# The order in which TensorE takes the columns of a matmul: groups of eight in place of groups of four, and the first block in that order too

## The chip, the cores and the metric

The kernel runs on one core of one Trainium2 chip. The metric is the device time of one execution in microseconds. Smaller is better.

## The reference, cut to what matters

Two sequences of 6080 tokens with 256 channels go through a gated scan and then through a feed-forward pair of products with an ELU between them.

```python
sig = 1 / (1 + exp(-f_logit))
f = lower_bound + (1 - lower_bound) * sig
for t in range(S):                       # S = 6080, for both batches
    h = f[:, t] * h + (1 - f[:, t]) * x[:, t]
    y[:, t] = h
hid = y.reshape(B * S, 256) @ w_in       # 256 -> 2048
g = where(hid > 0, hid, exp(min(hid, 0)) - 1)
out = g @ w_out                          # 2048 -> 256
```

All inputs and the output are float32.

## The kernel before, in words

**Layout.** Channels lie on the 128 partitions, tokens along the columns. The tokens of a sequence are cut into 12 blocks: block 0 has 448 columns (`SHORT`), blocks 1 to 11 have 512 (`TILE`). Both sequences are worked on in each block.

**Precision.** Each float32 operand is split into a rounded part and a rest, both of type float32r (`_hi`, `_lo`). Each product of two matrices is then three matmuls: hi with hi, hi with lo, lo with hi (lines 866 to 868 for the first layer, 897 to 899 for the second, 1002 to 1004 for the first layer in block 0).

**Work of TensorE.** In blocks 1 to 11 the first layer is done in seven products for each pair of hidden tiles instead of eight (a Strassen-like scheme; `P1` to `P7`, written out in `whole`, line 905). For each of the 8 pairs (`q`) a block has 7 products of three matmuls and 8 half tiles of the second layer of three matmuls: 45 matmuls, 360 in a block, 3960 in the eleven blocks. Block 0 uses the plain form: 32 tiles (`FIRST_TILES`), each with 6 matmuls of the first layer and 6 of the second, 384 in all. Before it stand 18 warm-up matmuls on bf16 zeros (line 1010). TensorE's queue is `first_products` (the first six tiles of block 0, line 961), then `first_product(t)` and `second(0, t - 6)` in turn (line 1012), then `whole` for each block.

**The other engines.** For each tile of the hidden layer ScalarE computes a negated relu of the bank (line 466) and an exponential (line 472), VectorE forms the ELU from the bank and that (line 719), ScalarE rounds it into `g_hi` (line 480), and GpSimd forms `g_lo` (line 336). The matmuls of the first layer write PSUM banks `h`; a bank is written again when the ELU of the tile before it in that bank is done (line 994 waits for `g_ready`). In blocks from 1 on ScalarE copies a bank (`fork`, line 458) and VectorE adds banks (lines 698, 705, 713) between products. The scan of the next block (lines 620, 628) and the splits of the weights in block 0 lie between these, in an order written out by hand (`spare`, `first_spare`, `early`, `late`). The SP queue loads and stores. Matmul number `t` of block 0's second layer comes six tiles after its first layer.

**The order of columns.** The function `in_order` (line 56) turns a view of the columns into four passes: the columns are cut into groups of `LINE` neighbours, and pass number a takes groups a, a + 4, a + 8 and so on (`APART` = 4). Output, moving operand and their partner in the product get the same order, so each column's result stands where it stood. `product` (line 860) uses it for every matmul of the first layer in blocks 1 to 11, `second` (line 870) for those of the second layer unless the block is block 0 (line 895). In block 0, `first_products` (lines 969, 976, 979, 983) and `first_product` (lines 1000 to 1004) read and write their columns in plain order. With `LINE` = 4 a pass over 512 columns is 32 groups of 4 columns (16 bytes) that start 16 columns (64 bytes) apart.

Of the kernel before, what the change touches and what calls it, by code (L numbers as in the profile page):

```python
# [21 lines left out]
SHORT = SEQ - (BLOCKS - 1) * TILE  # L22
# [5 lines left out]

EDGE = 8

LINE = 4
APART = 4

WIDE = 1
# [2 lines left out]
P1, P2, P3, P5, P6, P7, P4 = range(7)  # L37
# [15 lines left out]
PLACE = ((P1, P2), (P5, P4))  # L53


def in_order(columns):

    return columns.rearrange("p (b a c) -> p a b c", a=APART, c=LINE)


def width(j):
    return SHORT if isinstance(j, int) and j == 0 else TILE
# [18 lines left out]
def gated_scan_elu_ffn(nc, first_gate, forget_logit, value, w_in, w_out, out):  # L81
    ctx = ExitStack()
    with ctx:
# [51 lines left out]
        h = ctx.enter_context(nc.psum_tensor("h", [P, 4, TILE], F32))  # L135
# [50 lines left out]
        def first_bank(t):  # L186
            k = FIRST_BANK[t]
            return h[:, k] if k < TILES else acc[:, 1, k - TILES]
# [10 lines left out]
        def a_parts(par, product):  # L199
            if product == P4:  # L200
                return a4_hi[:, :], a4_lo[:, :]
            k = product
            return a_hi[:, par, k], a_lo[:, par, k]
# [655 lines left out]
        def _(pe):  # L859
# [10 lines left out]
            def second(j, t, half):  # L870

                w = width(j)
                first = isinstance(j, int) and j == 0
                if first:
                    b, unit = FIRST_TILES[t]
                    opens = unit == 0
                else:
                    b, unit = TILE_OF[t % TILES][0], 2 * (t // TILES) + TILE_OF[t % TILES][1]
                    opens = unit == b
                q, u = divmod(unit, 2)  # L880
                closes = unit == UNITS - 1 - b
                if half == 0:
                    if first:
                        pe.wait_ge(w_out_lo_ready[q], 1)
                    if opens and first and b == 1:

                        pe.wait_ge(g_ready, max(k for k in range(TILES * PAIRS) if FIRST_BANK[k] >= TILES) + 1)
                    if opens and not first:
                        pe.wait_ge(acc_copied, BATCH * HALVES * (j - 1) + HALVES * (b + 1))
                    pe.wait_ge(g_lo_ready, TILES * PAIRS * j + t + 1)  # L890
                cols = slice(half * P, (half + 1) * P)
                hi, lo = w_out_hi[:, q, u, cols], w_out_lo[:, q, u, cols]
                bank = acc[:, b, half, 0:w]
                g_h, g_l = g_hi[:, t % RING, 0:w], g_lo[:, t % RING, 0:w]
                if not first:
                    bank, g_h, g_l = in_order(bank), in_order(g_h), in_order(g_l)
                nc.tensor.matmul(bank, hi, g_h, start=opens, stop=False)  # L897
                nc.tensor.matmul(bank, hi, g_l, start=False, stop=False)  # L898
                done = nc.tensor.matmul(bank, lo, g_h, start=False, stop=closes)  # L899
                if half == 1:  # L900
                    done.then_inc(mm2_done, 1)
                elif closes:
                    done.then_inc(acc_half, 1)

            def whole(j, par):
                def m(q, back, i, half):

                    at = q - back
                    if at >= 0:
                        second(j, TILES * at + i, half)  # L910
                    else:
                        second(j - 1, TILES * (PAIRS + at) + i, half)
# [43 lines left out]
            def plain_weights(unit, half):  # L956
                p, u = divmod(unit, 2)
                k = QUARTER[half][u]
                return w_in_hi[:, p, k], w_plain_low[p][:, k]

            def first_products():

                pieces = [a_parts(0, PLACE[0][i]) for i in range(HALVES)]
                pe.wait_ge(zeros_ready, 3)
                for half in range(HALVES):
                    pe.wait_ge(a_hi_ready, half + 1)
                    for unit in range(OPEN):
                        pe.wait_ge(w_plain_hi_ready, unit // 2 + 1)
                        nc.tensor.matmul(first_bank(unit), plain_weights(unit, half)[0],  # L969
                                         pieces[half][0], start=half == 0, stop=False)  # L970
                for unit in range(OPEN):
                    w = TILE if unit < WIDE else SHORT
                    bank = first_bank(unit)[:, 0:w]
                    if unit == 0:
                        pe.wait_ge(a_lo_ready[P1], 1)
                    nc.tensor.matmul(bank, plain_weights(unit, 0)[0], pieces[0][1][:, 0:w], start=False, stop=False)
                    pe.wait_ge(w_plain_lo_ready[unit // 2], 1)
                    for half in range(HALVES):
                        nc.tensor.matmul(bank, plain_weights(unit, half)[1], pieces[half][0][:, 0:w],  # L979
                                         start=False, stop=False)  # L980
                    if unit == 0:
                        pe.wait_ge(a_lo_ready[P2], 1)
                    done = nc.tensor.matmul(bank, plain_weights(unit, 1)[0], pieces[1][1][:, 0:w],
                                            start=False, stop=True)
                    done.then_inc(done_of[unit % TILES], 1)

            def first_product(t):
                b, unit = FIRST_TILES[t]
                bank = first_bank(t)[:, 0:SHORT]
                pe.wait_ge(w_plain_lo_ready[unit // 2], 1)  # L990
                earlier = [k + 1 for k in range(t) if FIRST_BANK[k] == FIRST_BANK[t]]
                if earlier:
                    pe.wait_ge(g_ready, earlier[-1])
                for half in range(HALVES):
                    pe.wait_ge(a_lo_ready[PLACE[b][half]], 1)
                    hi, lo = plain_weights(unit, half)
                    a_h, a_l = [part[:, 0:SHORT] for part in a_parts(0, PLACE[b][half])]
                    if t == TILES * PAIRS - 2 and half == 0:

                        nc.tensor.matmul(h[:, 3], hi, a_parts(0, P5)[0], start=True, stop=False)  # L1000
                    else:
                        nc.tensor.matmul(bank, hi, a_h, start=half == 0, stop=False)  # L1002
                    nc.tensor.matmul(bank, hi, a_l, start=False, stop=False)  # L1003
                    done = nc.tensor.matmul(bank, lo, a_h, start=False, stop=half == 1)  # L1004
                done.then_inc(done_of[t % TILES], 1)
# [3 lines left out]
            for k in range(WARM_UP):  # L1009
                nc.tensor.matmul(h[:, k % 4, :], zeros[:, 0:P], zeros[:, 0:TILE], start=True, stop=True)  # L1010
            first_products()
            for t in range(OPEN, TILES * PAIRS):
                first_product(t)
                if t >= LEAD:
                    for half in range(HALVES):
                        second(0, t - LEAD, half)
# [46 lines left out]
```

## Time and profile before

| what | value |
|---|---|
| median of 3 runs | 976.56 us (976.37 to 976.63) |
| the profiled execution's own time | 976.51 us |
| its span (first to last instruction) | 974.6 us |
| TensorE matmul busy | 969.0 us, 99% |
| VectorE busy | 724.4 us, 74% |
| ScalarE busy | 790.7 us, 81% |
| GpSimd busy | 630.6 us, 65% |
| granted TensorE clock | full in every slice |
| chain that ended last | TensorE 99% |

The profile's duration of one matmul (about 384 ns at 512 columns) is longer than the time from its start to the start of the next, since matmuls are pipelined. The rate of TensorE is therefore read from the distance of starts, called the pace below.

### The profile page before, as it was taken

Reading aid. Unit: us, or ns where it says so; the run is one execution under the profiler, and the core shown is the slowest. Engines: PE = TensorE matmul, PEld = TensorE weight load, DVE = VectorE, ACT = ScalarE, POOL = GpSimd, SP = SyncE. Lnnn points to the kernel's source line nnn. Section 1 sums busy time; section 2 is a strip of 40 time slices with the busy share of each in tenths; the row PEclk is TensorE's granted clock in tenths of the full one; section 3 lists DMA queues with packets and bytes.
Section 4 is the critical chain, followed back from the end, with each engine's and each line's share of the span. In section 5 each row is a group of like instructions: output and inputs, shape, how many; then the busy total and the mean of one; then the engine's idle time right before and its main releaser. Section 6 shows DMA issues by size and latency. Waiting matters only on the chain.

```text
span 974.6 us, 15016 instructions
## 1 busy us (share of the span) xinstructions
PE 969.0 (99%) x4362; PEld 815.1 (84%) x4362; DVE 724.4 (74%) x916; ACT 790.7 (81%) x1424; POOL 630.6 (65%) x477
## 2 busy tenths in 40 slices
PE   9999999999999999999999999999999999999998
PEld 6998888888888888888888888888888888888887
DVE  6987876976886796697688679678758867956444
ACT  7988878878888887887887888788788788787775
POOL 2587796576667667557656755856775765676544
PEclk9999999999999999999999999999999999999999
DMA  7212012002101201100210210120021021001001
GB/s 269 67 32 93 0 34 65 34 1 77 54 1 54 76 1 43 54 32 2 74 54 0 65 65 0 45 67 17 22 64 43 0 75 54 0 0 46 1 1 44
DMA packets 23078, 42.02 MB, mean 43 GB/s; under 512 B 2560, under 2 KB 4096, under 8 KB 23040
## 3 DMA queue, kind: packets, MB, share of 16 engines
q1 hardware_dynamic: 22752, 41.10, 13.1%
q10 hardware_dynamic: 288, 0.46, 0.2%
q8 instruction: 18, 0.29, 0.1%
q14 instruction: 20, 0.16, 0.1%
HBM read 29.10 MB, written 12.45 MB: 43 GB/s over the span
## 4 chain that ended last, share of the span: by engine, by line
PE 99%; DMA 0%; DVE 0%; ACT 0%; issue 0%; DVEq 0%
PE acc L898 17%; PE acc L897 17%; PE acc L899 17%; PE h L868 14%; PE h L867 14%; PE h L866 14%; PE h L1004 1%; PE h L1003 1%; PE h L1002 1%; DMA opening<-first_gate 0%; PE h L969 0%; PE h L979 0%; PE acc L1002 0%; PE acc L1003 0%; PE acc L1004 0%; DVE x L628 0%
## 5 line engine op out<-in xcount | busy, mean ns | idle before, releaser
L336 POOL TENSOR_TENSOR g_lo<-e,g_hi 128x512 fp32r<-128x512 f32 (+1 forms) x384 | 517.3, 1357 | 338.0 <-ACT g_hi L480 337.0
L466 ACT ACTIVATE e<-h 128x512 f32<-128x512 f32 (+1 forms) x379 | 225.1, 594 | 138.5 <-PE h L868 109.9
L719 DVE SCALAR_TENSOR_TENSOR e<-e,h 128x512 f32<-128x512 f32 (+1 forms) x379 | 256.6, 677 | 70.5 <-ACT e L472 69.8
L897 PE MATMUL acc<-g_hi,w_out_hi 128*128 128x512 f32 (+1 forms) x768 | 293.7, 382 | 0.0
L898 PE MATMUL acc<-g_lo,w_out_hi 128*128 128x512 f32 (+1 forms) x768 | 293.7, 382 | 0.0
L899 PE MATMUL acc<-g_hi,w_out_lo 128*128 128x512 f32 (+1 forms) x768 | 293.7, 382 | 0.0
L472 ACT ACTIVATE e<-e 128x512 f32<-128x512 f32 (+1 forms) x384 | 241.4, 629 | 9.8 <-issue 1.4
L480 ACT CAST g_hi<-e 128x512 fp32r<-128x512 f32 (+1 forms) x384 | 232.2, 605 | 18.3 <-DVE e L719 18.3
L866 PE MATMUL h<-a_hi,w_in_hi 128*128 128x512 f32 x616 | 236.6, 384 | 0.0
L868 PE MATMUL h<-a_hi,w_in_lo 128*128 128x512 f32 x616 | 236.6, 384 | 0.0
L867 PE MATMUL h<-a_lo,w_in_hi 128*128 128x512 f32 x616 | 236.5, 384 | 0.0
L897 PEld LDWEIGHTS acc<-g_hi,w_out_hi 128*128 128x128 f32 x768 | 143.8, 187 | 26.5
L899 PEld LDWEIGHTS acc<-g_hi,w_out_lo 128*128 128x128 f32 x768 | 143.8, 187 | 26.5
L898 PEld LDWEIGHTS acc<-g_lo,w_out_hi 128*128 128x128 f32 x768 | 143.8, 187 | 26.5
L868 PEld LDWEIGHTS h<-a_hi,w_in_lo 128*128 128x128 f32 x616 | 115.3, 187 | 22.3
L867 PEld LDWEIGHTS h<-a_lo,w_in_hi 128*128 128x128 f32 x616 | 115.3, 187 | 22.2
L866 PEld LDWEIGHTS h<-a_hi,w_in_hi 128*128 128x128 f32 x616 | 115.3, 187 | 22.2
L713 DVE TENSOR_TENSOR h<-p,h 128x512 f32<-128x512 f32 x88 | 61.0, 693 | 73.0 <-PE h L868 72.8
L628 DVE TENSOR_TENSOR_SCAN x<-opening,carry,x 128x512 f32<-128x512 f32 (+1 forms) x48 | 102.2, 2129 | 0.1
L698 DVE COPY p<-h 128x512 f32<-128x512 f32 x88 | 59.7, 679 | 47.4 <-PE h L868 47.2
L705 DVE TENSOR_TENSOR h<-p,h 128x512 f32<-128x512 f32 x88 | 60.7, 690 | 34.9 <-PE h L868 33.9
L620 DVE SCALAR_TENSOR_TENSOR x<-opening,x 128x512 f32<-128x512 f32 (+1 forms) x48 | 56.3, 1172 | 0.1
(77 smaller groups left out, 560.3 us busy)
## 6 DMA issues: line engine op xcount, KB each, us to landing
opening<-forget_logit SPq DMA_DIRECT2D x44, 256.0 KB, 2.6
x<-value SPq DMA_DIRECT2D x44, 256.0 KB, 2.7
out<-out_sb SPq DMA_DIRECT2D x44, 256.0 KB, 2.0
w_in_raw<-w_in SPq DMA_DIRECT2D x8, 256.0 KB, 5.4
w_out_raw<-w_out SPq DMA_DIRECT2D x8, 256.0 KB, 6.7
out<-out_sb SPq DMA_DIRECT2D x4, 224.0 KB, 2.0
x<-value SPq DMA_DIRECT2D x3, 224.0 KB, 6.0
opening<-forget_logit SPq DMA_DIRECT2D x2, 224.0 KB, 6.0
```

The source lines that it names most:

```text
L336: nc.gpsimd.tensor_tensor(g_lo[:, t % RING, 0:w], e[:, t % TILES, 0:w], g_hi[:, t % RING, 0:w].bitcast(F32), ALU.subtract).then_inc(g_lo_r ...
L466: nc.scalar.activation(e[:, i, 0:w], bank_of(j, t)[:, 0:w], ACT.Relu, scale=-1.0).then_inc(r_ready, 1)
L472: nc.scalar.activation(e[:, t % TILES, 0:w], e[:, t % TILES, 0:w], ACT.Exp, scale=-1.0).then_inc(e_ready, 1)
L480: nc.scalar.copy(g_hi[:, t % RING, 0:w], e[:, t % TILES, 0:w]).then_inc(g_hi_ready, 1)
L628: nc.vector.tensor_tensor_scan(x[:, b, i, 0:w], gate[:, b, i, 0:w], x[:, b, i, 0:w], carry[:, b, i], ALU.mult, ALU.subtract).then_inc(scan ...
L719: nc.vector.scalar_tensor_tensor(e[:, t % TILES, 0:w], e[:, t % TILES, 0:w], -1.0, bank_of(j, t)[:, 0:w], ALU.add, ALU.max).then_inc(g_rea ...
L866: nc.tensor.matmul(into, hi, a_h, start=start, stop=False, skip_group_check=True)
L867: nc.tensor.matmul(into, hi, a_l, start=False, stop=False, skip_group_check=True)
L868: return nc.tensor.matmul(into, lo, a_h, start=False, stop=True, skip_group_check=True)
L897: nc.tensor.matmul(bank, hi, g_h, start=opens, stop=False)
L898: nc.tensor.matmul(bank, hi, g_l, start=False, stop=False)
L899: done = nc.tensor.matmul(bank, lo, g_h, start=False, stop=closes)
```

## The change

`LINE` goes from 4 to 8, so that a pass over 512 columns is 16 groups of 8 columns (32 bytes) that start 32 columns (128 bytes) apart. The condition in `second` goes, and every matmul of block 0 (448 columns, 14 groups in a pass, and those of 512 columns at its opening) gets the same order. Number, size and order of the instructions, the waits and the buffers stay as they are.

```diff
-LINE = 4
+LINE = 8
 APART = 4
...
                 g_h, g_l = g_hi[:, t % RING, 0:w], g_lo[:, t % RING, 0:w]
-                if not first:
-                    bank, g_h, g_l = in_order(bank), in_order(g_h), in_order(g_l)
+                bank, g_h, g_l = in_order(bank), in_order(g_h), in_order(g_l)
...
                     for unit in range(OPEN):
                         pe.wait_ge(w_plain_hi_ready, unit // 2 + 1)
-                        nc.tensor.matmul(first_bank(unit), plain_weights(unit, half)[0],
-                                         pieces[half][0], start=half == 0, stop=False)
+                        nc.tensor.matmul(in_order(first_bank(unit)), plain_weights(unit, half)[0],
+                                         in_order(pieces[half][0]), start=half == 0, stop=False)
                 for unit in range(OPEN):
                     w = TILE if unit < WIDE else SHORT
-                    bank = first_bank(unit)[:, 0:w]
+                    bank = in_order(first_bank(unit)[:, 0:w])
...
-                bank = first_bank(t)[:, 0:SHORT]
+                bank = in_order(first_bank(t)[:, 0:SHORT])
...
-                    a_h, a_l = [part[:, 0:SHORT] for part in a_parts(0, PLACE[b][half])]
+                    a_h, a_l = [in_order(part[:, 0:SHORT]) for part in a_parts(0, PLACE[b][half])]
                     if t == TILES * PAIRS - 2 and half == 0:
 
-                        nc.tensor.matmul(h[:, 3], hi, a_parts(0, P5)[0], start=True, stop=False)
+                        nc.tensor.matmul(in_order(h[:, 3]), hi, in_order(a_parts(0, P5)[0]), start=True, stop=False)
```

The moving operands of lines 976, 979 and 983 are wrapped in `in_order` in the same way.

## Rows read from the trace of the kernel before

**Rows 1.** The page: busy time, and the chain that ended last.

```profile
PE 969.0 (99%) x4362; PEld 815.1 (84%) x4362; DVE 724.4 (74%) x916; ACT 790.7 (81%) x1424; POOL 630.6 (65%) x477
PEclk9999999999999999999999999999999999999999
PE 99%; DMA 0%; DVE 0%; ACT 0%; issue 0%; DVEq 0%
```

**Rows 2.** Lines 866 and 899, first and last start; timeline of TensorE, blocks 1 to 11.

```profile
L866 PE MATMUL h<-a_hi,w_in_hi x616: 379/385/397, 80.7 to 963.9; 128*128 128x512 f32 x154
L899 PE MATMUL acc<-g_hi,w_out_lo x768: 358/382/390, 17.8 to 971.0; 128*128 128x512 f32 x176, 128*128 128x448 f32 x16
...
499.79 0.39 PE L898 MATMUL acc<-g_lo,w_out_hi 128*128 128x512 f32 x1
505.83 0.38 PE L867 MATMUL h<-a_lo,w_in_hi 128*128 128x512 f32 x1
```

**Rows 3.** Timeline of TensorE in block 0: start, us, instruction; then one matmul of 512.

```profile
52.70 0.36 PE L1002 MATMUL h<-a_hi,w_in_hi 128*128 128x448 f32 x1
57.97 0.37 PE L1004 MATMUL h<-a_hi,w_plain_lo 128*128 128x448 f32 x1
...
74.59 0.39 PE L1000 MATMUL h<-a_hi,w_in_hi 128*128 128x512 f32 x1
74.82 0.37 PE L1003 MATMUL h<-a_lo,w_in_hi 128*128 128x448 f32 x1
```

**Rows 4.** Timeline of TensorE: warm-up matmuls of 512 bf16 columns.

```profile
5.10 1.89 PE L1010 MATMUL h<-e 128*128 128x512 bf16 x8
6.61 0.38 PE L1010 MATMUL h<-e 128*128 128x512 bf16 x1
```

**Rows 5.** Timeline of TensorE at the opening, 512 columns in plain order.

```profile
10.80 0.62 PE L969 MATMUL acc<-a_hi,w_in_hi 128*128 128x512 f32 x2
11.26 0.39 PE L976 MATMUL h<-a_lo,w_in_hi 128*128 128x512 f32 x1
11.49 0.62 PE L979 MATMUL h<-a_hi,w_plain_lo 128*128 128x512 f32 x2
11.94 0.39 PE L983 MATMUL h<-a_lo,w_in_hi 128*128 128x512 f32 x1
12.17 0.36 PE L976 MATMUL h<-a_lo,w_in_hi 128*128 128x448 f32 x1
```

**Rows 6.** Timeline of TensorE where block 1 begins, six matmuls in four passes.

```profile
80.70 0.39 PE L866 MATMUL h<-a_hi,w_in_hi 128*128 128x512 f32 x1
82.07 0.36 PE L897 MATMUL acc<-g_hi,w_out_hi 128*128 128x448 f32 x1
```

**Rows 7.** Windows: PE, PEld, DVE, ACT, POOL busy (count), PEclk, DMA share, GB/s.

```profile
28.00:60.00 32.00, 32.00 (x160) 29.66 (x159) 29.63 (x39) 30.76 (x66) 20.07 (x15) 1.00 0.16 50
186.00:262.00 76.00, 76.00 (x342) 63.69 (x341) 57.23 (x72) 61.88 (x110) 50.66 (x38) 1.00 0.13 42
870.00:946.00 76.00, 76.00 (x342) 63.69 (x341) 39.10 (x59) 58.91 (x103) 42.09 (x33) 1.00 0.04 15
```

**Rows 8.** Groups by line, 16 to 80 us, ScalarE's relu: busy, mean, idle before.

```profile
L466 ACT ACTIVATE e<-h 128x448 f32<-128x448 f32 x24 | 12.9, 538 | 0.0
```

**Rows 9.** Timelines of VectorE and TensorE: an ELU and the matmul that takes its bank.

```profile
51.46 0.62 DVE L719 SCALAR_TENSOR_TENSOR e<-e,h 128x448 f32<-128x448 f32 x1 [0.42 <-ACT e L472]
...
65.85 0.61 DVE L719 SCALAR_TENSOR_TENSOR e<-e,h 128x448 f32<-128x448 f32 x1
67.30 0.36 PE L1002 MATMUL h<-a_hi,w_in_hi 128*128 128x448 f32 x1
```

**Rows 10.** Timelines in block 1: the sum into bank 3 and product P4 after it.

```profile
88.56 0.68 DVE L713 TENSOR_TENSOR h<-p,h 128x512 f32<-128x512 f32 x1
89.63 0.38 PE L866 MATMUL h<-a_hi,w_in_hi 128*128 128x512 f32 x1
```

**Rows 11.** Waits of the whole run: engine, line, whom for, total us, times, longest.

```profile
ACT e L466 <- PE h L868: 109.9, 231, 1.1
DVE h L713 <- PE h L868: 72.8, 68, 2.1
PE h L969 <- ACT a_hi L441: 1.1, 1, 1.1
```

More of the change, by code:

```diff
@@ L968, in first_products @@
                         pe.wait_ge(w_plain_hi_ready, unit // 2 + 1)
-                        nc.tensor.matmul(first_bank(unit), plain_weights(unit, half)[0],
-                                         pieces[half][0], start=half == 0, stop=False)
+                        nc.tensor.matmul(in_order(first_bank(unit)), plain_weights(unit, half)[0],
+                                         in_order(pieces[half][0]), start=half == 0, stop=False)
                 for unit in range(OPEN):
                     w = TILE if unit < WIDE else SHORT
-                    bank = first_bank(unit)[:, 0:w]
+                    bank = in_order(first_bank(unit)[:, 0:w])
                     if unit == 0:
                         pe.wait_ge(a_lo_ready[P1], 1)
-                    nc.tensor.matmul(bank, plain_weights(unit, 0)[0], pieces[0][1][:, 0:w], start=False, stop=False)
+                    nc.tensor.matmul(bank, plain_weights(unit, 0)[0], in_order(pieces[0][1][:, 0:w]),
+                                     start=False, stop=False)
                     pe.wait_ge(w_plain_lo_ready[unit // 2], 1)
                     for half in range(HALVES):
-                        nc.tensor.matmul(bank, plain_weights(unit, half)[1], pieces[half][0][:, 0:w],
+                        nc.tensor.matmul(bank, plain_weights(unit, half)[1], in_order(pieces[half][0][:, 0:w]),
                                          start=False, stop=False)
@@ L982, in first_products @@
                         pe.wait_ge(a_lo_ready[P2], 1)
-                    done = nc.tensor.matmul(bank, plain_weights(unit, 1)[0], pieces[1][1][:, 0:w],
+                    done = nc.tensor.matmul(bank, plain_weights(unit, 1)[0], in_order(pieces[1][1][:, 0:w]),
                                             start=False, stop=True)
```

## The prediction, made before the changed kernel was built

> **What bounds the kernel now.** I read the page first: matmuls are under way 99% of the span, the chain that ended last is 99% TensorE, and the granted clock is full throughout, the 2.4 GHz level [rows 1]. A busy matmul engine need not be at its peak, so the next view is the timeline, for the distance from start to start. Blocks 1 to 11: from the first start of line 866 to the last of line 899 is 971.0 - 80.7 = 890.3 us. That stretch holds 3989 distances, of which 30 belong to block 0's last matmuls (202.7 ns each, below): (890.3 - 6.1) / 3959 = **223.3 ns** for 512 columns in four passes. The short stretch agrees: 27 distances in 6.04 us, 223.7 ns [rows 2]. The windows show the same 342 matmuls in 76 us early and late, though VectorE is busy 57 us in the one and 39 us in the other [rows 7]. So the pace is TensorE's own, and no traffic of another engine sets it. Among the waits the others wait for TensorE; TensorE's own largest is 1.1 us at the start [rows 11]. The time is number of matmuls times pace, and a change of the access order acts on all of it.
>
> **What the pace consists of.** Three more orders can be read.
> - bf16, 512 columns, plain order: eight matmuls cover 1.89 us, the last 0.38, so seven distances are 1.51 us, 216 ns [rows 4]. That is what 512 columns take when the operand is half as wide. I use it as the floor.
> - float32r, 512 columns, plain order: three distances from 10.80 to 11.49 give 230 ns, three from 11.49 to 12.17 give 227 ns, and a lone one later gives 230 ns [rows 5, 3].
> - float32r, 448 columns, plain order (block 0): 26 distances from 52.70 to 57.97, 202.7 ns [rows 3]. The floor scaled to 448 is 189.0.
>
> So above the floor stand 11 to 14 ns in plain order, 7.3 ns in four passes of groups of four, and 13.7 ns for 448 columns. The order does matter, and TensorE has 7.3 ns a matmul left to win in blocks 1 to 11.
>
> **The change, part by part.** No instruction, wait, DMA or buffer is added or taken away, so nothing is queued behind anything new.
>
> (a) *Groups of eight in blocks 1 to 11*: 3960 matmuls by an unknown difference of pace. Bounds: down to the floor, 7.3 ns x 3960 = 29 us less; up to the slower plain reading, 230 - 223.3 = 6.7 ns, 27 us more, and beyond if a 128-byte step meets something that no row shows. Inside, the nearest rows are the order of four and plain order, and what counts is what their excess is charged for. With groups of four a matmul makes 128 hops of 64 bytes: 7.3 / 128 = 0.057 ns a hop. With groups of eight there are 64 hops, and 64 boundaries inside the groups, where the fourth column is followed by its neighbour. If those are free, the excess halves to 3.65 ns: pace 219.7, **14.5 us less**. I take this value, for two reasons. First, the excess of plain order does not grow with its boundaries: 448 columns have 112 groups of four and 13.7 ns, 512 have 128 and 11 to 14. Second, it is not fixed either: the same plain 512 columns go at 230 and at 227 ns, and the first six matmuls in four passes of block 1 go at (82.07 - 80.70) / 6 = 228 ns before the pace settles at 223.3 [rows 5, 6]. That looks like streams that fall together in a rhythm, which fewer and longer hops disturb less, not like a price on each neighbouring pair. The evidence is thin, and the chances say so.
>
> (b) *Block 0 in passes*: 367 matmuls of 448 columns. In groups of eight by the same arithmetic: 56 hops, 3.2 ns above 189.0, 192.2; 10.5 ns x 367 = 3.9 us. Most of it can't be had. ScalarE is busy 30.8 of 32 us there, and its relu never waits for TensorE [rows 7, 8]: it paces itself, and an ELU comes no earlier when the product does. The product that starts at 52.70 reuses a bank whose ELU ended at 51.46 + 0.62 = 52.08: 0.6 us of slack [rows 3, 9]. At 67.30 it is 67.30 - 66.46 = 0.8 us [rows 9]. By then 10.5 ns on 270 matmuls have asked for 2.8 us. So TensorE begins to wait in block 0, and gains 0.8 us plus what the last 66 matmuls give: at most 0.7, of which the first sums of block 1 take some back (VectorE's ends at 89.24, the product starts at 89.63, 0.4 us [rows 10]). Bounds 0.4 and 1.5; I take **0.8 us less**, in every case below but the last.
>
> (c) *The 17 plain matmuls of 512 columns* are 12 at the opening, which waits for its inputs [rows 11], four after them, and one late. A few ns each: nothing.
>
> (d) *Cover.* In blocks 1 to 11 ScalarE is busy 61.9 of 76 us and VectorE 57.2 [rows 7]; at 219.7 ns a stretch of 76 us becomes 74.8. The tightest chain shown has 0.4 us of slack, and nine matmuls lie between the product that it waits for and the one that waits for it: 33 ns less. No new wait.
>
> Sum, against the profiled execution's 976.5 us (the median is 976.56): 976.5 - 14.5 - 0.8 = **961.2 us**. With (a) between nothing and the floor this case covers 947 to 973.
>
> By the Trainium skill (SBUF — State Buffer, Specifications) SBUF is read in lines of 16 bytes, and two hits on a line are enough. Both orders read whole lines of four columns, so by it (a) would be nothing, which is the second case below.
>
> **The rivals.**
>
> *No change in pace.* A hop and an inner boundary cost the same, or only the four passes matter and not their grain. For it: 16 bytes may be the grain of the reader, which both orders keep whole. Against it: nothing but that an exact tie of two numbers is rare. Time: 976.5 - 0.8 = 975.7.
>
> *Slower: neighbouring groups of four cost more than a hop.* Place: between the fourth and fifth column of each group of eight, 64 places a matmul. Price from plain order: 11 to 14 ns over 127 boundaries, 0.087 to 0.11 ns. Pace: 216 + 64 x 0.057 + 64 x (0.087 to 0.11) = 225.2 to 226.7; 1.9 to 3.4 ns x 3960 = 7.5 to 13.5 us more. It decides as soon as such a boundary costs over the 0.057 ns of a hop. Time: about 976.5 + 10.5 - 0.8 = 986, between 983 and 990. For it: plain order, all neighbours, is the slowest order in the trace, and groups of eight lie one step towards it. Against it: the two reasons under (a).
>
> *As slow as plain order, or worse.* The advantage belongs to the 64-byte step alone. Pace 227 to 230 or over: 15 to 27 us more, and block 0 gains nothing: 991 to 1003. For it: nothing shows that a step of 128 bytes works like one of 64. Against it: two orders as different as plain and four passes are only 3% apart. The Trainium skill (PSUM — Partial Sum Buffer, Specifications) says that any non-contiguous pattern slows matmuls significantly, which would make block 0 slower too. The trace disagrees for blocks 1 to 11: 223.3 ns in passes, 227 to 230 in plain order [rows 2, 5].
>
> **How the numbers follow.** Faster pace 0.40, same pace 0.22, slower by the inner boundaries 0.24, as slow as plain order or worse 0.14. A measurement of this kernel tells about 0.2%, 2 us, from no change. So faster 0.40; within 0.2%, the same pace with its 0.8 us, 0.22; slower 0.24 + 0.14 = 0.38. The range runs from the floor, 976.5 - 29 - 0.8 = 947, to 992: it leaves out nearly all of the last case and the thin edges, under 2 in 10. The forecast's own range is 947 to 973.
>
> **What would show it right or wrong.** In the timeline of a middle block the distance of starts should be about 219.7 ns, alike for lines 866 to 868 and 897 to 899; 342 matmuls in a window of 76 us become about 348. In block 0 starts should be nearer than 202.7 ns until TensorE waits for an ELU (line 719) at lines 1002 to 1004, a wait that the trace has nowhere now, and block 1 should begin 0.4 to 1.5 us earlier than 80.70. A middle pace of 223 is the first rival, 225 to 227 the second, 227 or more the third. If TensorE waits in the middle blocks, the cover under (d) was misread.

## The result, and the profile after

| what | before | after |
|---|---|---|
| median | 976.59 us (976.37 to 976.63, 4 runs) | 961.85 us (961.61 to 965.07, 4 runs) |
| profiled execution, own time | 976.51 us | 962.05 us |
| its span | 974.6 us | 960.2 us |
| pace at 512 columns, blocks 1 to 11 | 223.3 ns | 220.0 ns |
| pace at 448 columns, block 0 | 202.7 ns | 193.3 ns |

The ratio is 0.9857, with a 95% interval of 0.9836 to 0.9878: 1.4% faster. One of the four runs after took 965.07 us, the others 961.61 to 962.05, and that one run makes most of the interval's width. Of the runs of the kernel before that stood beside the experiments one, at 0.753 of the full clock, took 1232.52 us and is left out everywhere. The page of the changed kernel, the lines that answer to [rows 1]:

```profile
PE 954.3 (99%) x4362; PEld 815.4 (85%) x4362; DVE 722.3 (75%) x916; ACT 790.1 (82%) x1424; POOL 628.8 (65%) x477
PEclk9999999999999999999999999999999999999999
PE 96%; ACT 2%; DVE 1%; issue 1%; POOL 0%; ACTq 0%; POOLq 0%
```

The busy shares hardly move, which shows how little they say here: TensorE was at 99% before and is at 99% now. What is new is that 3% of the chain lies on ScalarE and VectorE. Where, and how fast the rest goes, the timelines and windows tell. First the source view (first and last start) and the timeline of TensorE in a middle block, against [rows 2]; the changed kernel's lines 896 to 898 are lines 897 to 899 of before. Then two windows, against [rows 7].

```profile
L866 PE MATMUL h<-a_hi,w_in_hi x616: 380/382/382, 79.8 to 949.5; 128*128 128x512 f32 x154
L898 PE MATMUL acc<-g_hi,w_out_lo x768: 352/380/395, 17.9 to 956.6; 128*128 128x512 f32 x176, 128*128 128x448 f32 x16
```

```profile
300.10 0.38 PE L866 MATMUL h<-a_hi,w_in_hi 128*128 128x512 f32 x1
301.42 0.38 PE L896 MATMUL acc<-g_hi,w_out_hi 128*128 128x512 f32 x1
```

```profile
28.00:60.00 32.00, 31.56 (x160) 29.39 (x159) 29.57 (x39) 31.05 (x66) 20.00 (x15) 1.00 0.16 50
186.00:262.00 76.00, 76.00 (x347) 64.73 (x346) 58.57 (x74) 63.41 (x115) 49.68 (x38) 1.00 0.13 42
```

Six distances from 300.10 to 301.42 are 1.32 us, 220 ns. Block 1's first matmul starts at 79.8, the last of the kernel at 956.6: 876.8 us in place of 890.3, **13.5 us less**. In block 0 the timeline gives two things, a faster pace and four holes:

```profile
12.49 0.35 PE L975 MATMUL h<-a_lo,w_in_hi 128*128 128x448 f32 x1
45.91 0.48 PE L896 MATMUL acc<-g_hi,w_out_hi 128*128 128x448 f32 x1 [0.37 <-DVE w_out_lo L690]
49.33 0.38 PE L898 MATMUL acc<-g_hi,w_out_lo 128*128 128x448 f32 x1
49.78 0.45 PE L1002 MATMUL h<-a_hi,w_in_hi 128*128 128x448 f32 x1
50.06 0.37 PE L1003 MATMUL h<-a_lo,w_in_hi 128*128 128x448 f32 x1
50.27 0.36 PE L1004 MATMUL h<-a_hi,w_plain_lo 128*128 128x448 f32 x1
...
55.84 0.35 PE L1004 MATMUL h<-a_hi,w_plain_lo 128*128 128x448 f32 x1
58.16 0.35 PE L1004 MATMUL h<-a_hi,w_plain_lo 128*128 128x448 f32 x1
...
49.07 0.61 DVE L719 SCALAR_TENSOR_TENSOR e<-e,h 128x448 f32<-128x448 f32 x1
```

Twelve distances from 55.84 to 58.16 are 2.32 us, 193.3 ns. At 49.78 TensorE starts 0.45 us after its last start: the ELU of the tile that held the bank ended at 49.07 + 0.61 = 49.68. Two more such waits follow near 52.4 and 66.8; in all three TensorE starts 0.10 us after the ELU has ended. At 45.91 it waits for `w_out_lo`, the rest of the weights of the second layer (line 690). The matmuls of 448 columns begin at 12.49 (before 12.17 [rows 5], this execution's opening was 0.3 us later) and block 1 at 79.8: 67.3 us in place of 80.70 - 12.17 = 68.5, **1.2 us less**. Together 13.5 + 1.2 - 0.3 = 14.4, the difference of the two spans.

### The profile page after: what moved, and what is told of

Same layout as the page of the kernel before. It is cut to its first block, busy times and chain, and to the rows that moved or that the text cites. A ratio compares the mean times of both kernels' runs of the same rounds, so it can differ in the third digit from the quotient of the medians.

```text
span 960.2 us, 15016 instructions
## 1 busy us (share of the span) xinstructions
PE 954.3 (99%) x4362; PEld 815.4 (85%) x4362; DVE 722.3 (75%) x916; ACT 790.1 (82%) x1424; POOL 628.8 (65%) x477
## 4 chain that ended last, share of the span: by engine, by line
PE 96%; ACT 2%; DVE 1%; issue 1%; POOL 0%; ACTq 0%; POOLq 0%
PE acc L896 17%; PE acc L898 17%; PE acc L897 17%; PE h L868 14%; PE h L866 14%; PE h L867 14%; ACT e L472 1%; PE h L1010 1%; PE h L1002 1%; PE h L1004 1%; PE h L1003 1%; ACT e L466 1%; DVE x L628 0%; PE h L968 0%; ACT w_out_hi L505 0%
```

## The experiments

The theory on record charged the time above the floor to hops between groups. Its rivals were that neighbouring boundaries cost, or that the distance from group to group (64 or 128 bytes) is what counts; the expectations below call the last one the distance theory. Paces of experiments are read from one view, the window from 200 to 900 us: 700 us divided by the count of matmuls less 1.7 (the two at the edges are counted whole; a record is some 385 ns long). This reading is good to 0.1 ns. For the kernel before and after, first and second window:

```profile
200.00:900.00 700.00, 700.00 (x3136) 586.65 (x3135) 532.29 (x659) 571.39 (x1017) 457.89 (x342) 1.00 0.12 37
```

```profile
200.00:900.00 700.00, 700.00 (x3183) 596.12 (x3182) 534.52 (x667) 578.73 (x1030) 462.66 (x345) 1.00 0.12 38
```

That is 700 / 3134.3 = 223.3 and 700 / 3181.3 = 220.0 ns, as read above.

### The two halves of the change

The kernel before, with groups of eight; block 0 stays in plain order:

```diff
-LINE = 4
+LINE = 8
```

> Groups of eight in blocks 1 to 11 only, block 0 in plain order: separates the two halves of the change. If they add up as the changed kernel's trace has them (13.6 us from blocks 1 to 11, 0.9 us before block 1 begins), the pace of a middle block is 220.0 ns, block 1 begins near 80.7 us, TensorE waits for nothing in block 0, and the time is 962.9 us. If block 0's order is worth nothing, 961.9; if the three waits that came up in block 0 cost more than its faster pace gave, under 961.5.

Measured: 963.35 us, ratio 0.9862 (0.9844 to 0.9879). The source view of line 866 and the window:

```profile
L866 PE MATMUL h<-a_hi,w_in_hi x616: 380/382/407, 81.2 to 951.5; 128*128 128x512 f32 x154
```

```profile
200.00:900.00 700.00, 700.00 (x3183) 596.23 (x3182) 535.09 (x666) 578.83 (x1030) 463.13 (x346) 1.00 0.12 38
```

The middle pace is 220.0 ns. Block 1 begins at 81.2, 68.5 us after the first matmul of 448 columns, as before, and TensorE waits for nothing in block 0. So groups of eight in blocks 1 to 11 give 13.5 of the 14.7 us between the medians, and block 0's order the rest: the halves add up to within 0.5 us of the 962.9 expected.

The changed kernel, with groups of four; block 0 is in passes too:

```diff
-LINE = 8
+LINE = 4
```

> Groups of four everywhere, block 0 too. Blocks 1 to 11 keep 223.3 ns. For block 0 the price per hop says 189.0 + 112 x 0.057 = 195.4 ns for 448 columns; a fixed addition to every matmul, as groups of eight showed it (512 columns 220.0, 448 columns 193.3, both 6.7 ns over one column per cycle of 2.4 GHz), says for groups of four 10.0 ns over it, so 196.7. Either way TensorE runs into ELUs that are paced by ScalarE, block 1 begins 0.5 to 1.2 us earlier, and the time is 975.4 to 976.1 us.

Measured: **988.63 us**, ratio 1.0121 (1.0103 to 1.0139), 12 us slower than the kernel before, where 0.5 to 1.2 us faster was expected. Block 0 did what was expected (13 distances from 20.11 to 22.67, 197 ns, and block 1 begins at 80.0, 67.4 us after the first of 448 columns). But blocks 1 to 11, whose instructions are those of the kernel before to the last one, changed pace. The fences below are the timeline, source view of line 866 and window of this run:

```profile
20.11 0.36 PE L896 MATMUL acc<-g_hi,w_out_hi 128*128 128x448 f32 x1
22.67 0.36 PE L897 MATMUL acc<-g_lo,w_out_hi 128*128 128x448 f32 x1
```

```profile
L866 PE MATMUL h<-a_hi,w_in_hi x616: 380/385/399, 80.0 to 975.9; 128*128 128x512 f32 x154
```

```profile
200.00:900.00 700.00, 700.00 (x3089) 579.16 (x3089) 526.36 (x649) 564.86 (x1005) 452.74 (x337) 1.00 0.12 36
```

700 / 3087.3 = 226.7 ns, with TensorE busy in all 700 us. It doesn't wait; it streams slower. The same instructions have two steady paces, 223.3 and 226.7. It is no toss of a coin from run to run: four runs took 988.45 to 988.73 us, and six of the kernel before, beside them, 976.25 to 977.43.

### Whether reading or writing makes it

```diff
# read only: the moving operands keep in_order, every bank loses it
-                into = in_order(bank[:, 0:w])
+                into = bank[:, 0:w]
...
# write only: the banks keep in_order, every moving operand loses it
-                a_h, a_l = in_order(a_h[:, 0:w]), in_order(a_l[:, 0:w])
+                a_h, a_l = a_h[:, 0:w], a_l[:, 0:w]
```

The same was done in `second`, `first_products` and `first_product`. In both kernels a column's result no longer stands where the column was read, so the output is wrong and only the time is of use.

> Only the moving operand is read in the four passes of groups of eight; results are written to the bank in plain order, so each column's result stands at another place (the output is in another order, and at the opening columns mix). If the gain comes from how SBUF is read, the pace stays at 220.0 ns and 193.3 ns; if it comes from how PSUM is written, it goes back to that of plain order, 227 to 231 and 202.7. In between if both have a part.

> The mirror of the run before it: the bank is written in the four passes of groups of eight, the moving operand is read in plain order (again the columns change places). Read side: 227 to 231 ns and 202.7 ns. Write side: 220.0 and 193.3.

Measured: 961.78 us for reading alone and 989.75 us for writing alone. The windows, reading first:

```profile
200.00:900.00 700.00, 700.00 (x3183) 596.11 (x3182) 534.25 (x667) 578.68 (x1031) 462.76 (x345) 1.00 0.12 38
```

```profile
200.00:900.00 700.00, 700.00 (x3090) 579.59 (x3090) 527.37 (x648) 564.97 (x1004) 454.86 (x338) 1.00 0.12 36
```

Reading alone has 220.0 ns, all of the gain; writing alone has 226.7 ns. The order in which PSUM is written is worth nothing: with groups of eight read, 220.0 ns whichever way the bank is written. The second run also gives what plain reading at 512 columns settles at: 226.7 ns, the lower of the two values in [rows 5]. No kernel that also writes in plain order was run, so this one stands for plain reading below.

### Group size and distance

```diff
-LINE = 8
+LINE = 16
```

The other three have `LINE = 4` with `APART = 8`, `LINE = 8` with `APART = 2`, and `LINE = 8` with `APART = 8`.

> Groups of 16, every fourth group, in all blocks (64 bytes in a group, 256 bytes from group to group, 32 hops in 512 columns). Price per hop (0.057 ns over a floor of 216): 217.8 ns and a time near 953. Run length (a run of 32 bytes is enough) : 220.0 ns, time 962. Plain-like (long runs bring back the plain order): towards 226.7, time up to 989. Distance theory (128 bytes or more from group to group is what counts): 220.0 or less.

> Groups of four, every eighth group: 16 bytes in a group as in the kernel before, 128 bytes from group to group as in the changed one, still 128 hops. Price per hop and run length: 223.3 to 226.7 ns (as groups of four had it), time 975 to 989. Distance theory: 220.0 ns, time 962.

> Groups of eight, every second group: 32 bytes in a group as in the changed kernel, 64 bytes from group to group as in the kernel before, 64 hops. Price per hop and run length: 219.7 to 220.0 ns, time 962. Distance theory: 223.3 to 226.7 ns, time 975 to 989.

> Groups of eight, every eighth group: eight passes, 256 bytes from group to group, 64 hops. Price per hop, run length and distance theory all say 220.0 ns and 962 us; if instead the number of passes costs something (a fixed price at each return to the start, four cycles of 2.4 GHz a pass as 16 cycles over 512 would have it), 32 cycles over 512, 226.7 ns and 989 us.

The windows of these four, in this order:

```profile
200.00:900.00 700.00, 700.00 (x2924) 554.43 (x2923) 510.26 (x618) 535.27 (x951) 426.81 (x317) 1.00 0.12 36
```

```profile
200.00:900.00 700.00, 700.00 (x2840) 546.90 (x2839) 494.27 (x599) 520.11 (x922) 415.27 (x310) 1.00 0.11 36
```

```profile
200.00:900.00 700.00, 700.00 (x3014) 565.82 (x3013) 521.20 (x636) 550.85 (x979) 440.49 (x329) 1.00 0.12 36
```

```profile
200.00:900.00 700.00, 700.00 (x3002) 591.00 (x3001) 520.23 (x635) 549.38 (x975) 439.33 (x327) 1.00 0.11 36
```

| group, apart | bytes in a group | bytes to the next | hops | pace, ns | time, us |
|---|---|---|---|---|---|
| plain reading (written in passes of eight) | all | | 0 | 226.7 | 989.75 |
| 4, 4 (block 0 plain) | 16 | 64 | 128 | 223.3 | 976.59 |
| 4, 4 (block 0 too) | 16 | 64 | 128 | 226.7 | 988.63 |
| 8, 4 | 32 | 128 | 64 | **220.0** | **961.85** |
| 16, 4 | 64 | 256 | 32 | 239.5 | 1042.26 |
| 4, 8 | 16 | 128 | 128 | 246.6 | 1071.73 |
| 8, 2 | 32 | 64 | 64 | 232.4 | 1013.57 |
| 8, 8 | 32 | 256 | 64 | 233.3 | 1018.77 |

The rows of plain reading, of 4, 8 and of 8, 2 are one run each, the others four. Sixteen with four apart has a ratio of 1.0672 (1.0654 to 1.069), eight with eight apart 1.0432 (1.0415 to 1.045). Every account on record falls. The price per hop wanted the fastest pace from 16 and 4, and one and the same from the three orders with 64 hops; they have 220.0, 232.4 and 233.3. The distance theory wanted 220 from 4 and 8, which is the slowest of all. A run of 32 bytes is not enough either. Only a price per pass foresaw that eight passes of eight are slower, and its 226.7 ns is well under the 233.3 measured. Four of the six orders in passes are slower than plain order.

### Moving the operands against the weights

By now one code had two steady values of the pace, the order of writing had no part in it, and none of the properties of the read order in the table explained it. TensorE reads one other thing from SBUF in this trace: the next weights are loaded beside each matmul (PEld in the page). The next runs therefore move the moving operands in SBUF and leave the weights where they are.

```diff
-        sb("room_of_edge", [P, P - EDGE])
+        sb("room_of_edge", [P, P - EDGE + 16])   # 64 bytes; + 8 for 32 bytes
```

> The changed kernel with gates, x, a_hi, a_lo, e, g_hi and g_lo (the moving operands among them) 64 bytes further in SBUF, the weights of blocks 1 to 11 where they were. If the time lost in a matmul comes from the moving operand's reads meeting the reads of the next weights, the relative place of the two counts and the pace of a middle block leaves 220.0 ns (anything from 216 to 247, as other orders showed). If the moving stream's own order alone makes it, 220.0 ns and 962 us stay.

> The same with 32 bytes, a quarter of the 128 bytes from group to group, so that each group of eight stands in the place of its neighbour. Weights theory: another pace than 220.0 ns, and not that of 64 bytes either unless the place repeats every 32 bytes. Own order alone: 220.0 ns and 962 us.

Measured: 988.61 and 1007.95 us, one run each. The window for 64 bytes, a stretch of the same run's timeline, and the window for 32 bytes:

```profile
200.00:900.00 700.00, 700.00 (x3090) 581.02 (x3089) 525.88 (x649) 564.36 (x1005) 452.12 (x337) 1.00 0.12 36
```

```profile
299.98 0.39 PE L866 MATMUL h<-a_hi,w_in_hi 128*128 128x512 f32 x1
300.21 0.39 PE L867 MATMUL h<-a_lo,w_in_hi 128*128 128x512 f32 x1
300.44 0.38 PE L868 MATMUL h<-a_hi,w_in_lo 128*128 128x512 f32 x1
300.66 0.39 PE L896 MATMUL acc<-g_hi,w_out_hi 128*128 128x512 f32 x1
```

```profile
200.00:900.00 700.00, 700.00 (x3030) 568.92 (x3029) 520.98 (x638) 553.65 (x984) 444.74 (x332) 1.00 0.12 36
```

700 / 3088.3 = 226.7 ns and 700 / 3028.3 = 231.2 ns, with the same order of columns, the same instructions and nothing idle. In the first, the matmul at line 868, during which the weights of another product are fetched, takes 0.22 us to the next start, the two before it 0.23. Over the whole window of the trace, in nanoseconds, it is 219 against 231 and 230; with the shift of 32 bytes it is 233.3 after lines 867 and 868 and 226.7 after line 866. In the kernels before and after, each line has the same mean distance.

Two readings were left: the place against the weights, or the place as such (some boundary in SBUF that a group now straddles). One run tells them apart by moving all tiles.

```diff
-        sb("room_before", [P, -base % 512], mybir.dt.uint8)
+        sb("room_before", [P, -base % 512 + 64], mybir.dt.uint8)
```

> The changed kernel with every tile, weights and moving operands alike, 64 bytes further in SBUF. If the 6.7 ns that moving the operands alone by 64 bytes added (226.7 in place of 220.0) came from their place against the weights, it is gone: 220.0 ns, 962 us. If it came from where the operands themselves start (a line or row of SBUF that a group of eight now straddles), it stays: 226.7 ns, 988 us.

Measured: 961.84 us in one run. The window:

```profile
200.00:900.00 700.00, 700.00 (x3183) 596.23 (x3182) 534.28 (x667) 578.80 (x1031) 462.46 (x345) 1.00 0.12 38
```

220.0 ns again. It is the place of the moving operands relative to the tiles that stayed, and of these TensorE reads only the weights. A third reading is that a shift changes block 0 and so only how the stream comes in (next section). Against it: the first 36 distances of 448 columns, right behind the opening, already go at 196.7 ns with 64 bytes and 203.8 with 32, where the kernel after and the run with all tiles moved have 193.3 and 193.4; and groups of eight, four apart, unshifted, settled at 220.0 ns whether block 0 was in passes or plain. No run excludes it for blocks 1 to 11.

### Whether the way in decides the pace

```diff
# changed kernel; product() and second() of blocks 1 to 11 with groups of four
-                into = in_order(bank[:, 0:w])
+                into = in_order(bank[:, 0:w], 4)
...
+                line = LINE if first else 4
```

> Groups of eight in block 0, groups of four in blocks 1 to 11, whose instructions are then those of the kernel before and of the run with groups of four everywhere. Those two ran at 223.3 and 226.7 ns. If the pace in blocks 1 to 11 depends on how the stream comes in (its phase at the end of block 0), this run lands on one of these two, or on a third value, and keeps it to the end: about 974 or 987 us. If block 0 had only held those matmuls back by a wait in them, TensorE would show idle time in blocks 1 to 11.

Measured: 988.16 us in one run, and the window has 3090 matmuls, 226.7 ns:

```profile
200.00:900.00 700.00, 700.00 (x3090) 579.19 (x3089) 526.80 (x648) 564.79 (x1004) 452.51 (x338) 1.00 0.12 36
```

So with either order in passes in block 0 the groups of four settle at 226.7 ns, and with plain order there they settle at 223.3, and each keeps its pace to the end. TensorE is busy through the whole window, so no pause breaks the stream. The kernel before stands on the better of the two paces seen.

The starts in the trace, taken in nanoseconds, show what settles: the distances run through a fixed cycle. In a middle block the kernel before repeats every four matmuls (224, 221, 219, 230), groups of four with block 0 in passes every seven (225, 226, 220, 221, 221, 234, 239), the changed kernel every two (219, 221), the one shifted by 64 bytes every three (219, 231, 230), and plain reading stands at 226 or 227. So three runs that share the mean of 226.7 ns do so by different cycles. Groups of four have a cycle of four and one of seven, and which they fall into is decided by what came before. What in block 0 decides it, its order or the waits that come with that order (in the run with groups of four everywhere the starts at line 1002 near 49.9 and 52.6 us come 0.4 us after the last, while the kernel before has no such gap), was not separated.

## Why the prediction was right, and where it was not

**Direction and size.** 961.2 us was forecast, 961.85 measured. Step by step:

- *The pace sets the time, and no other engine has a hand in it.* Right. Blocks 1 to 11 gave 13.5 us: (223.3 - 220.0) x 3960 = 13.1 us by the rounded paces, 13.3 by the starts in nanoseconds, and 0.3 from the 30 matmuls of 448 columns that stand among the first of block 1 (202.6 against 193.3 ns).
- *(a) A hop costs 0.057 ns, inner boundaries nothing, hence 219.7 ns.* The number was near, 220.0; **the reasoning behind it was wrong**. Groups of sixteen, with half the hops, should have come to 217.8 and came to 239.5; two other orders with 64 hops came to 232.4 and 233.3. Even inside the changed kernel the price per hop misses: it wanted 192.2 ns for 448 columns, and the pace is 193.3. The remark that carried it, that the pace looks like streams falling together in a rhythm and not like a price on each boundary (the same plain columns at 230 and 227 ns), is what the experiments bear out. But a rhythm gives no right to a linear price. The rows of before left anything from 216 ns upwards open, and plain reading, 230 ns, was no upper bound for an order in passes: four of those tried lie above it, up to 246.6. That 8 and 4 came out 0.3 ns from the forecast, and the time 0.65 us from it, was luck; the direction had a chance of 0.40 on record.
- *(b) Block 0 gains 0.8 us, between 0.4 and 1.5, since ScalarE paces it.* 1.2 us measured. The waits for ELUs at line 1002 came in three places, two of them those whose slack the prediction had read (0.6 and 0.8 us). The wait for `w_out_lo` at 45.9 was missed: only the slack of the banks had been read, not that of the weights of the second layer. It cost about 0.6 us (0.75 us from start to start in place of 0.19). After each wait the next start comes after 0.28 to 0.32 us. Behind the waits at 49.78 and 66.79 ten or more matmuls then go at 197 to 210 ns (50.06 to 50.27 is one of them), behind the other two only one goes over 200. Without the holes 367 x (202.7 - 193.3) = 3.4 us would have been gained.
- *(c) The 17 plain matmuls are worth nothing.* Nothing shows otherwise; the opening's own jitter of 0.3 us is larger.
- *(d) No new wait in blocks 1 to 11.* Right: TensorE is busy in all of the 700 us of its window.

**The rivals.** *No change in pace*, by a 16-byte grain of reading, is refuted by 220.0 against 223.3 in the same plain-block-0 setting. The Trainium skill's line of 16 bytes (SBUF — State Buffer, Specifications) may hold, but it does not decide the pace: 16, 4 and 8, 4 both take whole lines and are 19.5 ns apart. *Inner boundaries cost more than hops* is refuted by the same 220.0 ns, where it asked for over 223.3; and groups of four, eight apart, which have no inner boundaries, are slowest. *The advantage belongs to the 64-byte step* is refuted too: the best order steps by 128 bytes, and 8, 2 with a step of 64 has 232.4 ns. The Trainium skill's rule that any non-contiguous pattern slows matmuls (PSUM — Partial Sum Buffer, Specifications) does not show on the PSUM side at all: the bank written in passes or in plain order gives the same 220.0 ns. On the side of SBUF, against plain reading at 226.7 ns, four orders are slower, 8, 4 is faster (220.0), and 4, 4 is faster (223.3) or equal (226.7).

**What is shown and what is not.** Shown: the difference between 220.0 ns and plain reading arises where TensorE reads the moving operand from SBUF; the pace changes when that operand moves against the tiles that stay; and for one code it can settle at more than one value. Argued only: that the weights are the tile that counts, and that the two reads, of columns and of the next weights, meet in the same part of SBUF. What makes the 6.7 ns that even the best order takes above 512 cycles at 2.4 GHz is open as well. No run took the weight loads away, and which address bits collide was not found; the paces in the table fit no rule that I could state. Whether some other pair of group and distance, or another offset, comes closer to 216 ns was not tried beyond these runs.

## What to carry to other kernels

Where TensorE is busy without a gap, read the distance of starts and compare it with a lone stream of the narrower type; what stands above may be the order and place of the operands, and no rule found here foretells it: of six orders in passes one was better than plain by 3%, one by 1.5% or nothing, four were worse, and a shift of 32 bytes cost 5%. Treat group, distance and the offset between weights and moving tiles as one setting, try them together, and measure again after any edit that moves a tile or changes the stream ahead, since the same instructions can settle at another pace. Shifting all tiles alike by 64 bytes was harmless.

## What the runs showed of the hardware that I had not expected

- A matmul of 512 float32r columns takes 220.0 to 246.6 ns in steady state by the order of reading alone, and 220.0, 226.7 or 231.2 ns by an offset of 0, 64 or 32 bytes between moving operands and weights. bf16 in plain order takes 216 ns [rows 4].
- Identical instructions ran at 223.3 or 226.7 ns through all of blocks 1 to 11 (some 890 or 900 us), by what block 0 had been, in repeating cycles of four or of seven distances.
- In groups of eight four apart, 448 and 512 columns both take 6.7 ns more than as many cycles at 2.4 GHz would (193.33 - 186.67 and 220.0 - 213.3), while in plain order the shorter matmul has the larger excess (202.7 - 186.7 = 16.0 against 226.7 - 213.3 = 13.4).
